# v's feature-major copy comes from memory, and only u is turned on the chip by a product with half an identity

## The chip, the cores and the metric

One core of one Trainium2 chip runs the whole program. The metric is the device time of one execution in microseconds (us). The engines are TensorE (PE, with its weight loads as PEld), VectorE (DVE), ScalarE (ACT), GpSimd (POOL) and SyncE (SP), which here issues all DMAs.

## What is computed

Inputs r, k, v, w, a, b of shape (4, 8, 768, 40), float32: 4 sequences, 8 heads, 768 time steps, 40 features. A state of 40 x 40 per head runs over time, and two dense layers follow on its 3072 x 320 outputs:

```
for t in range(S):
    y[:, :, t] = einsum('bhd,bhde->bhe', rt, state)
    Sa = einsum('bhde,bhe->bhd', state, at)
    state_decay = state * wt[:, :, None, :] - einsum('bhd,bhe->bhde', Sa, bt)
    state = state_decay + einsum('bhd,bhe->bhde', vt, kt)
x = (sigmoid(x @ w_gate) * (x @ w_val)) @ w_out          # x: y as 3072 x 320; hidden 1536
out = max(x @ w1, x @ w2, x @ w3) @ w_out2               # hidden 768
```

## The kernel before

**The recurrence.** Time is cut into 12 "pairs" (k = 0 to 11) of 64 steps. The heads stand in 12 slots of up to three heads (120 rows of features), in three groups g = 0, 1, 2 of four slots each: two parities (par) by two positions (pos). Groups 0 and 1 have slots of three heads (hd = 120), group 2 of two (hd = 80). Within a pair the updates of the state are solved as a triangular system: the grams of a (`ga`, six a pair, u = 2g + par) give its matrix, GpSimd inverts it for two pairs at once (`solve_block`, L385 to L400), and products with the inverse give u, the corrections of v. The tile `vu_rows` holds v and u with time on partitions: for each parity 64 rows of v at 64 * (1 - par) and 64 rows of u at 64 * par. From it come the state's increment (L495), and the grams of r (`gr`, L561), whose masked form (`gr_m`) times `kb_rows` gives y (L579).

The grams of r need v and u with features on partitions. That is the step `vt` (`turn_vu`, L517 to L525): four transposes a group on TensorE through the helper at L414 (all transposes stand under L415), each of 128 rows by hd columns, into the bank `p_tr`, which `ts` (the state) and `kb` also use in turn; ScalarE copies the result to `vu_t` (`keep_vu`, L804; all its copies stand under L752) and signals `tr_kept`.

**The order.** Every engine walks the same list of steps, `TURN` (L51 to L61), one turn a pair, with the pairs shifted against one another: in turn t, PE works on the solve of pair t, the outputs (`vt`, `gr`, `y`) of pair t - 1 and the grams of a of pair t + 3. In a turn the steps that matter here come in this order on PE:

```
vx 0, ga 0, ty 2, vt 0, ga 1, vx 1, t1 0, ga 2, ts 0, gr 0, ga 3, vx 2, t1 1, low 0, ga 4, gr 1, vt 1,
ga 5, y 0, t1 2, low 1, t2 0, gr 2, ts 1, ty 0, gr 3, low 2, t2 1, inc 0, vt 2, y 1, t2 2, kb 0, inc 1,
gr 4, ts 2, ty 1, gr 5, kb 1, inc 2, y 2, kb 2
```

Turns run from -4 to 13; `vt` stands in turns 1 to 12, `ga` in turns up to 8. The grams of a use one bank from pair 4 on, so each `ga` waits for VectorE's mask (`mask_a`, L667) of the one ahead; likewise each `gr` for `mask_r` (L676). In every even turn up to 8 VectorE turns the blocks of two pairs for the solve (`lab`, L682, behind `gr 2`), and at the end of every odd turn it turns the inverse (`inv`, L688), which it can do when GpSimd has finished; both stand in its order with everything else.

**The transfers.** SP issues every DMA in an order written out in its own `turn` (L280): in turn k the load of `r_m` (L265; r of one group, masked by head) for group 2 of pair k - 1, for group 0 and then group 1 of pair k, each behind the grams that used its buffer two groups before; the stores of y (L274, L277); and the loads of w, a, kb, v, r. Behind turn 11 SP first issues the loads of the next layer (`gated.load_x`, `gated.load_weights`, L881 to L949) and only then turn 12, with the last `load_rm(11, 2)`. The next layer begins when all engines have met at the end of the block.

**The two layers** behind it are dense products on TensorE (L875, L1045, L1260), each float32 operand split in a high and a low part.

Of the kernel before, what the change touches and what calls it, by code (L numbers as in the profile page):

```python
# [21 lines left out]
PT = 2 * C  # L22
PAIRS = SEQ // PT
SLOTS = 12
E3 = 120
# [4 lines left out]
GO = (0, 240, 480)  # L30
# [88 lines left out]
    return ap.broadcast_to(shape)  # L119


def recurrence(nc, w_in, a_in, kb_in, r_in, rm_in, v_in, x1_out, gated):
    ctx = ExitStack()
    with ctx:
        def sb(name, shape, dt=F32):
            return ctx.enter_context(nc.sbuf_tensor(name, shape, dt))

        def sem(name):
            return ctx.enter_context(nc.semaphore(name))
# [16 lines left out]
        a_m = sb("a_m", [E3, 2, 4, 3 * PT])  # L146
        r_t = sb("r_t", [E3, 2, SLOTS, PT])
        r_m = sb("r_m", [E3, 2, 4, 3 * PT])
        vu_t = sb("vu_t", [E3, 2, 4, 128])
        kb_rows = sb("kb_rows", [128, 5, 2, ROWS])  # L150
        vu_rows = sb("vu_rows", [128, 3, 2, ROWS])
        ak = sb("ak", [128, 4, 2, 16, PT])
# [14 lines left out]
        ld_w_first = sem("ld_w_first")  # L167
        ld_a = [sem(f"ld_a{x}") for x in range(5)]
        ld_v = [sem(f"ld_v{x}") for x in range(3)]
        ld_w, ld_kb, ld_r, ld_rm, st_y = ([sem(f"{n}{x}") for x in range(2)]  # L170
                                          for n in ("ld_w", "ld_kb", "ld_r", "ld_rm", "st_y"))
        consts = sem("consts")
        prod_done = sem("prod_done")
        ends_done = sem("ends_done")
# [35 lines left out]
        def w_of(k):  # L210

            if k == 1:
                return s_rows[:, :, :, :].rearrange("e z s f -> e (z s f)")[:, 0:4 * SLOTS * SEG].rearrange(
                    "e (z f) -> e z f", z=2)
            return w_raw

        def gram_bank(k, u):

# [7 lines left out]
        def _(sp):  # L226
# [33 lines left out]
            def load_rm(k, g):  # L260
                n = 3 * k + g
                if n >= 2:
                    sp.wait_ge(gr_done, 2 * (n - 2) + 2)
                rows, cols = HD[g], HPS[g] * PT
                sp.dma_start(r_m[0:rows, n % 2, :, 0:cols],  # L265
                             rm_in[k, 0:rows, 4 * g:4 * g + 4, 0:cols]).then_inc(ld_rm[n % 2], 16)

# [143 lines left out]
        def _(pe):  # L411
            mm = nc.tensor.matmul

            def turn(out, in_):  # L414
                return nc.tensor.transpose(out, in_, ident[0:in_.shape[0], 0:in_.shape[0]])  # L415
# [101 lines left out]
            def turn_vu(k, g):  # L517
                hd = HD[g]
                tr_free("vt", k, g)
                for par in range(2):  # L520
                    for pos in range(2):
                        at = 2 * par + pos
                        last = turn(p_tr[0:hd, at * 128:at * 128 + 128],
                                    vu_rows[:, k % 3, par, GO[g] + pos * hd:GO[g] + pos * hd + hd])
                last.then_inc(tr_done, 1)  # L525

            def turn_y(k, g):
# [23 lines left out]
            def gram_r(k, u):  # L551
                g, par = divmod(u, 2)
                n, hd, cols = 3 * k + g, HD[g], HPS[g] * PT
                if par == 0:
                    pe.wait_ge(tr_kept, TR_USE["vt", k, g] + 1)
                    pe.wait_ge(ld_rm[n % 2], 16 * (n // 2) + 16)
                pe.wait_ge(grm_done, 6 * k + u)
                if k == 0 and u == 0:
                    pe.wait_ge(akm_done, 24)
                for pos in range(2):  # L560
                    last = mm(p_gr[:, pos * cols:pos * cols + cols], vu_t[0:hd, n % 2, 2 * par + pos, :],  # L561
                              r_m[0:hd, n % 2, 2 * par + pos, 0:cols], start=pos == 0, stop=True,
                              skip_group_check=True)
                last.then_inc(gr_done, 1)
# [185 lines left out]
        def _(act):  # L750
            def copy(out, in_, scale=1.0):
                return nc.scalar.activation(out, in_, ACT.Copy, scale=scale)  # L752
# [51 lines left out]
            def keep_vu(k, g):  # L804
                n, hd = 3 * k + g, HD[g]
                act.wait_ge(tr_done, TR_USE["vt", k, g] + 1)
                if n >= 2:
                    act.wait_ge(gr_done, 2 * (n - 2) + 2)
                copy(vu_t[0:hd, n % 2, :, :], p_tr[0:hd, :].rearrange("e (s f) -> e s f", s=4)).then_inc(tr_kept, 1)

            def keep_y(k, g):
                n = 3 * k + g
# [559 lines left out]
            run_block(BLOCKS - 1, 1, False)  # L1372


def program(nc, w_in, a_in, kb_in, r_in, rm_in, v_in, w_gate, w_val, w_out, m_w1, m_w2, m_w3, m_out, out):
    x1 = nc.dram_tensor("x1", (BLOCKS, DM, BATCH, TB), F32).ap()
    with ExitStack() as ctx:

        lent_x = ctx.enter_context(nc.sbuf_tensor("lent_x", [128, 2 * SLOTS * 2 * SEG], F32))
        lent_w = ctx.enter_context(nc.sbuf_tensor("lent_w", [128, 2 * SLOTS * 128], F32))  # L1380
        gated = GatedInputs(nc, ctx, x1, w_gate, w_val, w_out, lent_x, lent_w)
        recurrence(nc, w_in, a_in, kb_in, r_in, rm_in, v_in, x1, gated)
        x2 = ctx.enter_context(nc.sbuf_tensor("x2", [128, BLOCKS, KT, TOK], F32))
        weights = MaxWeights(nc, ctx, (m_w1, m_w2, m_w3), m_out, lent_w)
        gated_layer(nc, gated, x2, weights)
        max_layer(nc, x2, weights, out.rearrange("(b n t) f -> n t b f", b=BATCH, n=BLOCKS))


def lay_out(r, k, v, w, a, b):
    def by_feature(x, pad):  # L1390
        out = np.full((PAIRS, E3, SLOTS, PT), pad, np.float32)
        for s, (bt, j) in enumerate(SLOT_HEADS):
            hs = x[bt, 3 * j:3 * j + 3]
            rows = hs.shape[0] * D
            out[:, 0:rows, s] = hs.reshape(-1, PAIRS, PT, D).transpose(1, 0, 3, 2).reshape(PAIRS, rows, PT)
        return out

    ws = by_feature(w, 1.0).reshape(PAIRS, E3, SLOTS, 2, C)
    w33 = np.zeros((PAIRS, E3, 2, SLOTS, 2, SEG), np.float32)
    w33[:, :, 0, :, :, 1:] = ws  # L1400
    w33[:, :, 1, :, :, 1:] = ws[..., ::-1]

    kf, bf = by_feature(k, 0.0), by_feature(b, 0.0)
    kb = np.zeros((PAIRS, E3, SLOTS, 2, PT), np.float32)
    rf = by_feature(r, 0.0)
    rm = np.zeros((PAIRS, E3, SLOTS, 3, PT), np.float32)
    vr = np.zeros((PAIRS, 2, PT, ROWS), np.float32)
    for s, (bt, j) in enumerate(SLOT_HEADS):
        g, par, pos = s // 4, s // 2 % 2, s % 2
        kb[:, :, s, 1 - par] = kf[:, :, s]  # L1410
        kb[:, :, s, par] = bf[:, :, s]
        for i in range(3):
            rm[:, i * D:(i + 1) * D, s, i] = rf[:, i * D:(i + 1) * D, s]
        hs = v[bt, 3 * j:3 * j + 3]
        cols = hs.shape[0] * D
        at = GO[g] + pos * HD[g]
        vr[:, par, :, at:at + cols] = hs.reshape(-1, PAIRS, PT, D).transpose(1, 2, 0, 3).reshape(PAIRS, PT, cols)
    return {
        "w_in": w33.reshape(PAIRS, E3, 2, SLOTS * 2 * SEG),
        "a_in": by_feature(a, 0.0),  # L1420
        "kb_in": kb.reshape(PAIRS, E3, SLOTS, 2 * PT),
        "r_in": rf,
        "rm_in": rm.reshape(PAIRS, E3, SLOTS, 3 * PT),
        "v_in": vr,
    }


# [15 lines left out]
```

## Time and profile before

| | us |
|---|---|
| median of 3 runs | 1127.23 |
| lowest, highest | 1122.25, 1128.94 |
| the profiled execution | 1123.35 |
| its span, first to last instruction | 1121.6 |
| PE busy in the span | 1039.6 (93%) |
| DVE, ACT, POOL busy | 514.6, 352.0, 291.3 |
| mean granted clock of TensorE | 0.954 of full speed |

A row of the timeline is a start, a length, the engine, the line, what was written from what, and how many instructions were merged; in brackets the idle time before it and what ended it. Granted clock 1.0 is 2.4 GHz, 0.5 is 1.2 GHz.

### The profile page before, as it was taken

The numbers are of one execution on the slowest core, as the hardware profiler recorded it, in microseconds if no ns is written. First come the engines' busy times: TensorE is split into PE (matmuls) and PEld (weight loads), VectorE is DVE, ScalarE is ACT, GpSimd is POOL, SyncE is SP. The second block draws the span as 40 slices with busy tenths as digits, with TensorE's granted clock in tenths as the row PEclk, the third lists the DMA queues.
The fourth block names the chain that finished last, engine by engine and source line by source line (L and its number), as shares of the span: only waits on it lengthen the run. The fifth ranks groups of instructions, "written<-read, shape, count | busy, mean of one in ns | idle before, by whom it ended". The sixth has DMA issues, their size and how long they took to land. (4 is left out here: it accounts for less than half of the span.)

```text
span 1121.6 us, 21667 instructions
## 1 busy us (share of the span) xinstructions
PE 1039.6 (93%) x8872; PEld 867.0 (77%) x8872; DVE 514.6 (46%) x875; ACT 352.0 (31%) x732; POOL 291.3 (26%) x527
## 2 busy tenths in 40 slices
PE   6577999899989996999999999999997999999998
PEld 3445778787778885788888888888885888888886
DVE  6726776567774443553323223332225543342432
ACT  3213544444444442432222222222223211111111
POOL 4788869588785500000000000000000000000000
PEclk7766999899999998899999999999998999999999
DMA  7632345455522225630000200000002100000000
GB/s 173 157 78 68 94 112 136 95 135 131 125 71 71 72 65 136 177 97 0 29 1 23 60 1 1 1 0 0 0 0 64 45 24 23 1 24 8 16 23 23
DMA packets 53247, 66.23 MB, mean 59 GB/s; under 512 B 19944, under 2 KB 40680, under 8 KB 53160
## 3 DMA queue, kind: packets, MB, share of 16 engines
q1 hardware_dynamic: 53160, 65.00, 22.7%
q8 instruction: 63, 1.03, 0.4%
q14 instruction: 24, 0.20, 0.1%
HBM read 57.12 MB, written 7.86 MB: 58 GB/s over the span
## 5 line engine op out<-in xcount | busy, mean ns | idle before, releaser
L1144 DVE TENSOR_TENSOR hid<-gate,gbank 128x512 f32<-128x512 f32 x72 | 49.5, 688 | 204.1 <-ACT gate L1090 204.1
L875 PE MATMUL mbank<-x_hi,w_hi 128*128 128x512 f32 x324 | 127.7, 394 | 6.7 <-DVE w_lo L1329 6.7
L392 POOL TENSOR_TENSOR inv_step<-lab 128x30 f32<-128x30 f32 (+9 forms) x180 | 120.0, 667 | 35.9 <-DVE lab L682 22.2
L875 PE MATMUL mbank<-x_hi,w_lo 128*128 128x512 f32 x324 | 127.0, 392 | 0.0
L1090 ACT ACTIVATE gate<-gbank 128x512 f32<-128x512 f32 x72 | 43.1, 598 | 226.4 <-PE gbank L875 226.4
L400 POOL TENSOR_TENSOR lab<-lab,inv_step 128x30 f32<-128x30 f32 (+9 forms) x180 | 110.4, 613 | 14.1
L1346 DVE TENSOR_TENSOR hid<-hid,mbank 128x512 f32<-128x512 f32 x72 | 49.5, 687 | 97.3 <-PE mbank L875 94.2
L875 PE MATMUL gbank<-x_hi,g_hi 128*128 128x512 f32 x216 | 84.9, 393 | 8.0 <-DVE v_lo L1124 8.0
L875 PE MATMUL mbank<-x_lo,w_hi 128*128 128x512 f32 x216 | 85.3, 395 | 0.0
L1045 PE MATMUL gbank<-h_hi,o_hi 128*128 128x512 f32 x216 | 84.1, 390 | 1.0 <-DVE h_lo L1150 1.0
L875 PE MATMUL gbank<-x_hi,g_lo 128*128 128x512 f32 x216 | 84.8, 392 | 0.0
L875 PE MATMUL gbank<-x_hi,v_hi 128*128 128x512 f32 x216 | 84.3, 391 | 0.0
L875 PE MATMUL gbank<-x_hi,v_lo 128*128 128x512 f32 x216 | 84.3, 390 | 0.0
L1045 PE MATMUL gbank<-h_lo,o_hi 128*128 128x512 f32 x216 | 84.0, 389 | 0.0
L546 PE MATMUL bank<-a_m,lent_w 120*128 120x192 f32 (+1 forms) x288 | 66.8, 371 | 18.2 <-DVE lent_w L657 10.9
L875 PEld LDWEIGHTS mbank<-x_hi,w_hi 128*128 128x128 f32 x324 | 61.5, 190 | 19.1 <-issue 7.1
L1150 DVE TENSOR_TENSOR h_lo<-hid,h_hi 128x512 fp32r<-128x512 f32 x72 | 49.9, 692 | 49.1 <-ACT h_hi L1095 49.1
L546 PEld LDWEIGHTS bank<-a_m,lent_w 120*128 120x128 f32 (+1 forms) x288 | 52.7, 224 | 24.7 <-issue 14.3
L875 PEld LDWEIGHTS mbank<-x_hi,w_lo 128*128 128x128 f32 x324 | 61.5, 190 | 13.2
L561 PE MATMUL bank<-r_m,vu_t 120*128 120x192 f32 (+1 forms) x288 | 59.5, 330 | 10.3 <-DVE gr_m L676 8.1
L752 ACT ACTIVATE b_sb<-bank 32x240 f32<-32x240 f32 x144 | 48.8, 339 | 63.3 <-PE bank L439 44.8
L374 POOL COPY lab_rows<-ak 32x192 f32<-32x192 f32 (+1 forms) x144 | 55.4, 384 | 40.6 <-DVE ak L667 34.6
(130 smaller groups left out, 2015.0 us busy)
## 6 DMA issues: line engine op xcount, KB each, us to landing
lent_w<-kb_in SPq DMA_DIRECT2D x12, 720.0 KB, 6.7
r_m<-rm_in SPq DMA_DIRECT2D x24, 360.0 KB, 3.7
lent_x<-w_in SPq DMA_DIRECT2D x10, 742.5 KB, 6.1
a_t<-a_in SPq DMA_DIRECT2D x12, 360.0 KB, 4.7
r_t<-r_in SPq DMA_DIRECT2D x11, 360.0 KB, 6.6
vu_rows<-v_in SPq DMA_DIRECT2D x24, 160.0 KB, 6.1
out<-o_sb SPq DMA_DIRECT2D x6, 640.0 KB, 3.2
x<-y_t SPq DMA_DIRECT2D x48, 60.0 KB, 3.2
```

The lines of the kernel that those rows point to most:

```text
L374: last = nc.gpsimd.tensor_copy(lab_rows[at:at + C, lane:lane + nh, :], ak[at:at + C, k % 4, par, HO[g]:HO[g] + nh, C * half:C * half + C])
L392: product = nc.gpsimd.tensor_tensor(part, column, row, op=ALU.mult)
L400: step(nc.gpsimd.tensor_tensor(rest, rest, part, op=ALU.subtract))
L546: last = mm(gram_bank(k, u)[:, pos * cols:pos * cols + cols], kb_t[0:hd, k % 2, slot_of(g, par, pos), :], a_m[0:hd, n % 2, 2 * par + pos, ...
L561: last = mm(p_gr[:, pos * cols:pos * cols + cols], vu_t[0:hd, n % 2, 2 * par + pos, :], r_m[0:hd, n % 2, 2 * par + pos, 0:cols], start=pos ...
L752: return nc.scalar.activation(out, in_, ACT.Copy, scale=scale)
L875: last = mm(out, w, x, start=n == 0, stop=n == len(seq) - 1)
L1045: last = nc.tensor.matmul(p_out[t][:, :], w, h, start=m == 0 and n == 0, stop=m == M1 - 1 and n == len(seq) - 1)
L1090: nc.scalar.activation(gate[:, m % 2, :], p_gate[m % 2][:, :], ACT.Sigmoid).then_inc(gate_done, 1)
L1144: nc.vector.tensor_tensor(hid[:, m % 2, :], gate[:, m % 2, :], p_val[m % 2][:, :], op=ALU.mult).then_inc(hid_done, 1)
L1150: nc.vector.tensor_tensor(h_lo[:, m % 2, :], hid[:, m % 2, :], h_hi[:, m % 2, :].bitcast(F32), op=ALU.subtract).then_inc(hl_done, 1)
L1346: nc.vector.tensor_tensor(hid[:, n, m % 2, :], hid[:, n - 1, m % 2, :], bank_of(b, m, n)[:, :], op=ALU.max).then_inc(most, 1)
```

## The change

The host gives v a second time, as `vt_in`, in the layout by features that a and r have. SP loads of it, ahead of each load of `r_m` and behind the same wait, the two slots of each parity straight into `vu_t`, where v's half of the 128 columns lies: 2 loads a group, 72 in all, of 120 (or 80) rows by 2 runs of 256 bytes. On TensorE `turn_vu` no longer transposes all 128 rows. It takes an ordinary product of the same weights (128 rows by hd columns of `vu_rows`) with 64 columns of the identity, those of u's rows, so that 64 columns come out; ScalarE copies 4 x 64 columns instead of 4 x 128 into u's places in `vu_t`. The grams of r wait for the two loads too (`ld_vt`). `vu_t` grows from 512 to 640 elements a buffer so that one slice can name u's places of both parities.

```diff
-        vu_t = sb("vu_t", [E3, 2, 4, 128])
+        vu_t = sb("vu_t", [E3, 2, 5 * 128])
...
+        def vu_slots(n, par):
+
+            return vu_t[:, n % 2, 256 * par:256 * par + 256].rearrange("e (o t) -> e o t", o=2)
...
                 if n >= 2:
                     sp.wait_ge(gr_done, 2 * (n - 2) + 2)
                 rows, cols = HD[g], HPS[g] * PT
+                for par in range(2):
+                    at = slot_of(g, par, 0)
+                    sp.dma_start(vu_slots(n, par)[0:rows, :, 64 * (1 - par):64 * (1 - par) + 64],
+                                 vt_in[k, 0:rows, at:at + 2, :]).then_inc(ld_vt[n % 2], 16)
                 sp.dma_start(r_m[0:rows, n % 2, :, 0:cols],
                              rm_in[k, 0:rows, 4 * g:4 * g + 4, 0:cols]).then_inc(ld_rm[n % 2], 16)
...
                 for par in range(2):
                     for pos in range(2):
                         at = 2 * par + pos
-                        last = turn(p_tr[0:hd, at * 128:at * 128 + 128],
-                                    vu_rows[:, k % 3, par, GO[g] + pos * hd:GO[g] + pos * hd + hd])
+                        last = mm(p_tr[0:hd, at * PT:at * PT + PT],
+                                  vu_rows[:, k % 3, par, GO[g] + pos * hd:GO[g] + pos * hd + hd],
+                                  ident[:, 64 * par:64 * par + 64], start=at == 0, stop=True, skip_group_check=True)
                 last.then_inc(tr_done, 1)
...
                     pe.wait_ge(ld_rm[n % 2], 16 * (n // 2) + 16)
+                    pe.wait_ge(ld_vt[n % 2], 32 * (n // 2) + 32)
...
-                    last = mm(p_gr[:, pos * cols:pos * cols + cols], vu_t[0:hd, n % 2, 2 * par + pos, :],
+                    last = mm(p_gr[:, pos * cols:pos * cols + cols], vu_slots(n, par)[0:hd, pos, :],
...
-                copy(vu_t[0:hd, n % 2, :, :], p_tr[0:hd, :].rearrange("e (s f) -> e s f", s=4)).then_inc(tr_kept, 1)
+                u_part = vu_t[0:hd, n % 2, :].rearrange("e (p x) -> e p x", p=2)[:, :, 0:256].rearrange(
+                    "e p (o x) -> e p o x", o=2)[:, :, :, 0:PT]
+                copy(u_part, p_tr[0:hd, 0:4 * PT].rearrange("e (p o x) -> e p o x", p=2, o=2)).then_inc(tr_kept, 1)
...
+        "vt_in": by_feature(v, 0.0),
```

## Rows read from the trace of the kernel before

**Rows 1.** Busy time by stretches of 40 us: PE, PEld, DVE, ACT, POOL, clock, DMA.

```profile
280.00:320.00 40.00, 36.91 (x656) 31.20 (x655) 27.64 (x55) 19.02 (x48) 31.11 (x48) 1.00 0.43 103
...
560.00:1121.00 561.00, 548.64 (x2556) 463.19 (x2554) 194.48 (x275) 129.38 (x216) 0.00 (x0) 0.99 0.06 17
```

**Rows 2.** Timeline of VectorE, the turns of lower blocks and inverse, 283 to 387 us.

```profile
284.12 1.94 DVE L682 STREAM_TRANSPOSE lab<-lab_rows 128x1024 f32<-128x1024 f32 x1
...
330.91 1.97 DVE L688 STREAM_TRANSPOSE inv_rows<-lab 128x1024 f32<-128x1024 f32 x1 [1.19 <-POOL lab L400]
...
346.52 1.93 DVE L682 STREAM_TRANSPOSE lab<-lab_rows 128x1024 f32<-128x1024 f32 x1
...
383.38 1.95 DVE L688 STREAM_TRANSPOSE inv_rows<-lab 128x1024 f32<-128x1024 f32 x1
```

**Rows 3.** Timeline of PE in turn 12, grams of group 2.

```profile
438.01 0.68 PE L561 MATMUL bank<-r_m,vu_t 80*128 80x128 f32 x4 [1.36 <-issue]
```

**Rows 4.** Timeline of SP's queue, turns 11 and 12.

```profile
425.30 0.35 SPq L265 DMA_DIRECT2D r_m<-rm_in  x1
425.69 0.90 SPq L274 DMA_DIRECT2D x<-y_t  x2
...
427.20 1.18 SPq L941 DMA_DIRECT2D lent_x<-x  x2
...
429.06 2.35 SPq L883 DMA_DIRECT2D lent_w<-moe_w_gate  x2
...
434.55 0.61 SPq L265 DMA_DIRECT2D r_m<-rm_in  x1
...
446.19 0.41 SPq L881 DMA_DIRECT2D x<-moe_w_gate  x1
```

**Rows 5.** PE's groups by shape, 0 to 450 us: busy us, mean ns, idle.

```profile
L579 PE MATMUL bank<-kb_rows,gr_m 128*64 128x40 f32 x768 | 28.6, 228 | 0.1
L495 PE MATMUL bank<-vu_rows,kb_rows 128*120 128x120 f32 x176 | 23.4, 276 | 4.0 <-DVE s_t L703 3.2 <-issue 0.7
...
L415 PE MATMUL bank<-ident,vu_rows 128*80 128x128 f32 x48 | 7.2, 273 | 0.0
...
L415 PE MATMUL bank<-ident,s_t 80*80 80x80 f32 x44 | 4.8, 233 | 0.0
```

**Rows 6.** Timeline of PE about "vt 0" and "vt 1".

```profile
300.73 0.60 PE L415 MATMUL bank<-ident,vu_rows 128*120 128x128 f32 x4
301.42 0.89 PE L546 MATMUL bank<-a_m,lent_w 120*128 120x192 f32 x4
...
310.75 0.60 PE L415 MATMUL bank<-ident,vu_rows 128*120 128x128 f32 x4
311.19 0.61 PE L546 MATMUL bank<-a_m,lent_w 80*128 80x128 f32 x4
```

**Rows 7.** Timeline of PE, the products used as prices.

```profile
318.73 1.00 PE L495 MATMUL bank<-vu_rows,kb_rows 128*120 128x120 f32 x8
...
320.56 0.85 PE L579 MATMUL bank<-kb_rows,gr_m 128*64 128x40 f32 x24
...
329.53 0.50 PE L415 MATMUL bank<-ident,lent_w 80*128 80x80 f32 x4 [0.88 <-ACT kb_rows L752]
```

**Rows 8.** ScalarE's groups by shape: busy us, mean ns, idle.

```profile
L752 ACT ACTIVATE vu_t<-bank 120x512 f32<-120x512 f32 x24 | 14.3, 597 | 21.6 <-PE bank L415 21.5
L752 ACT ACTIVATE y_rows<-bank 128x240 f32<-128x240 f32 x24 | 8.9, 370 | 18.8 <-PE bank L579 18.8
```

**Rows 9.** Timeline of a usual turn: r_m of group 2 issued, then used.

```profile
310.95 0.34 SPq L265 DMA_DIRECT2D r_m<-rm_in  x1
...
323.86 0.62 PE L561 MATMUL bank<-r_m,vu_t 80*128 80x128 f32 x4
```

**Rows 10.** DMA issues: count, KB each, us from issue to landing.

```profile
r_m<-rm_in SPq DMA_DIRECT2D x24, 360.0 KB, 3.7
```

**Rows 11.** Busy time in one stretch, columns as in rows 1.

```profile
207.00:214.00 7.00, 7.00 (x57) 6.09 (x54) 1.51 (x3) 2.44 (x6) 2.36 (x8) 0.52 0.35 73
```

More of the change, by code:

```diff
@@ L119, in bc, with recurrence @@
     return ap.broadcast_to(shape)
-def recurrence(nc, w_in, a_in, kb_in, r_in, rm_in, v_in, x1_out, gated):
+def recurrence(nc, w_in, a_in, kb_in, r_in, rm_in, v_in, vt_in, x1_out, gated):
     ctx = ExitStack()
@@ L169, in recurrence @@
         ld_v = [sem(f"ld_v{x}") for x in range(3)]
-        ld_w, ld_kb, ld_r, ld_rm, st_y = ([sem(f"{n}{x}") for x in range(2)]
-                                          for n in ("ld_w", "ld_kb", "ld_r", "ld_rm", "st_y"))
+        ld_w, ld_kb, ld_r, ld_rm, ld_vt, st_y = ([sem(f"{n}{x}") for x in range(2)]
+                                          for n in ("ld_w", "ld_kb", "ld_r", "ld_rm", "ld_vt", "st_y"))
         consts = sem("consts")
@@ L1372, in _, with program @@
             run_block(BLOCKS - 1, 1, False)
-def program(nc, w_in, a_in, kb_in, r_in, rm_in, v_in, w_gate, w_val, w_out, m_w1, m_w2, m_w3, m_out, out):
+def program(nc, w_in, a_in, kb_in, r_in, rm_in, v_in, vt_in, w_gate, w_val, w_out, m_w1, m_w2, m_w3, m_out, out):
     x1 = nc.dram_tensor("x1", (BLOCKS, DM, BATCH, TB), F32).ap()
@@ L1381, in program @@
         gated = GatedInputs(nc, ctx, x1, w_gate, w_val, w_out, lent_x, lent_w)
-        recurrence(nc, w_in, a_in, kb_in, r_in, rm_in, v_in, x1, gated)
+        recurrence(nc, w_in, a_in, kb_in, r_in, rm_in, v_in, vt_in, x1, gated)
         x2 = ctx.enter_context(nc.sbuf_tensor("x2", [128, BLOCKS, KT, TOK], F32))
```

## The prediction

> **What bounds the kernel now.** I read the page first (one core, TensorE, called PE, is the busiest engine), then the table by stretches of 40 us [rows 1]. The change touches only the recurrence, which ends near 446 us; behind 560 us PE is busy for 548.6 of 561 us, at a granted clock of 0.99, in the two layers that the diff leaves alone. Inside the recurrence PE is busy for 92% of a middle stretch (280 to 320), but a busy share does not say which wait sets the pace, so I looked in the timeline for waits that close a loop.
>
> There is one. In every second turn VectorE turns the inverse for two pairs (L688), and it stands idle before it until GpSimd has finished its solve (L400): 1.19 us at 330.91 [rows 2], and waits of the same kind stand in turns 2, 4 and 6. The solve can start only when VectorE has turned the lower blocks (L682, at 284.12 and 346.52), and from the end of that turn (284.12 + 1.94 = 286.06) to L688 GpSimd needs 44.8 us [rows 2]. So a period of two turns, 346.52 - 284.12 = 62.4 us, has two parts. From L682 to L688, 46.8 us, GpSimd sets the pace, and PE has 1.19 us to spare. From L688 to the next L682, some 15.6 us, PE does. After 346.52 nothing more is solved for later: L688 at 383.38 stands without idle, PE is in front to the end, and its work counts in full.
>
> The last stretch is different again. In turn 12 PE stands still for 1.36 us before the grams of group 2 (438.01) [rows 3] and the releaser is "issue", which is no engine. Before that the queue of SP works through a backlog: from 425.30 to 435 one transfer follows another, because the loads of the next layer stand between the loads of r_m. The last r_m is issued at 434.55 and PE goes on 3.46 us later [rows 3, 4]. I read this as the wait for that transfer.
>
> **What the change removes, adds and moves.** There are 36 steps "vt" (12 pairs by 3 groups). Each was four transposes of all 128 rows of vu_rows, and becomes four products with 64 columns of the identity.
>
> *PE.* The transposes of group 2 have 48 records, one for each of 12 x 4 [rows 5]. An ordinary float32 product leaves two: L495 has 176 records at groups 0 and 1, where the program has 11 x 2 x 4 = 88 products [rows 5]. So the four new products are eight passes of 64 columns, against four of 128: the same number of columns. The pitch of a transpose is (600 - 273) / 3 = 109 ns (four in 0.60 us, one lasting 273 ns) [rows 5, 6], so a step is 436 ns now. For a product pass of 120 columns, eight in 1.00 us give (1000 - 276) / 7 = 103 ns [rows 5, 7]; that is 0.86 ns a column, 55 ns for 64. Is the weight load hidden beneath 55 ns? At L579, 24 passes take 0.85 us, two by two in two halves of the array: (850 - 228) / 23 = 27 ns each, 54 ns for a pair that loads 2 x 64 = 128 columns and streams only 40 [rows 5, 7]. So 54 ns are a load of about 128 columns, and 120 columns hide just under the stream. With two to spare I take 57 ns, 8 x 57 = 456 ns, 20 ns more than now. Below, 53 ns (8 x 53 = 424, 12 ns less); above, the 4 turns of 80 columns with weights 128 wide, which take at most (500 - 233) / 3 = 89 ns each [rows 5, 7]: 8 x 89 = 712, 276 ns more. The row nearest in width and kind is L495, which is why I stay low.
>
> The Trainium skill, "TensorE: Matmul & The Clock Gate", section "LDWEIGHTS (loading the stationary operand)", prices a load at its columns over 1.2, so 100 ns for 120 columns; each step would then be an estimated 8 x 100 = 800 ns. The trace disagrees: 54 ns for 128 columns at L579.
>
> Which steps count? "vt 0" of turns 1 to 8 is followed by a gram of a that waits for the mask of the gram ahead; PE is idle there: four transposes from 300.73 have streamed at 300.73 + 0.44 = 301.17, and the next product starts at 301.42 [rows 6]. 20 ns vanish in those 0.25 us. "vt 1" (310.75) is followed at once, 0.44 us later, by the next gram (311.19) [rows 6], and "vt 2" by outputs, so they move PE. But only what lies between L688 and L682 (vt 1 of turns 2, 4, 6, 8: 4 steps) or behind the last L682 (vt 2 of turn 8 and three steps in each of turns 9 to 11: 10 steps) moves the end. The rest is taken from PE's 1.19 us to spare. 14 x 0.020 = +0.28 us; at the two ends 14 x (-0.012) = -0.2 and 14 x 0.276 = +3.9 us.
>
> *ScalarE.* The copy of a step goes from 512 to 256 elements a row. 597 ns for 512 and 370 for 240 from PSUM [rows 8] are 0.83 ns an element, so 383 ns: 214 ns less, 36 times. Nothing waits for it until turn 12: after "vt" PE uses the same bank again only two or more steps later, and the grams that read vu_t come turns or half turns on. In turn 12 the first gram does wait for it, but what that gains stands before the 1.36 us of idle and is lost in them. Worth nothing.
>
> *The transfers.* 72 loads of 60 or 40 KB in runs of 256 bytes; the stores of y have that shape and cost SP 0.45 us each (two in 0.90) [rows 4]. In a usual turn there is cover: r_m of group 2 is issued at 310.95 and used at 323.86 [rows 9], 12.9 us for two more issues (0.9) and 3.7 us of landing [rows 10]. If that cover went, "gr" would wait and y behind it. The added wait itself (PE on ld_vt) is one more semaphore among four on the same step and ends before the gram is due.
>
> Not so in turn 12. Each load of r_m now has two loads of v ahead of it on SP, and SP is the one that is late. Two stand at 425.30, behind the last gram of turn 11 that frees the buffer: 0.85 us, the first short issue (0.35) and one of the usual. Two more stand before 434.55 in the backlog, where two short transfers take 1.18 us [rows 4]: 1.2 us. Together 2.05 us, by which the last r_m lands later, counted from the end of turn 11. PE waits for it already, so it all goes to the end: y of the last group, its turn, its store, and the next layer, which starts when all engines have met (SP's first load there at 446.19) [rows 4]. Bounds: 4 x 0.33 = 1.3 us if each cost the shortest issue shown (0.35), 3.2 us if the backlog stalls once more as at 429.06 (2.35 for two instead of 1.18).
>
> **The sum.** 0.28 + 2.05 = +2.3 us. Against the profiled span, 1121.6 + 2.3 = 1123.9 us. That execution took 1123.35 us in all, 1.75 more than its span, and the median of the runs is 1127.23, their spread 6.7 us. So I predict 1127.2 + 2.3 = 1129.5 us. What a measurement of this kernel can tell from no change is about 1%, 11.3 us.
>
> **The rivals.**
> *The last r_m is not what PE waits for, or SP's extra issues hide.* For it: "issue" names no transfer. Against it: nothing else of that step is late. Then +0.3 us: 1127.5.
> *The clock gains.* PE's granted clock falls to 0.52 (about the lower level, 1.2 of 2.4 GHz) from 207 to 214 us and is back at 1.00 behind it [rows 11]. That stretch lies behind L688, where PE counts. At half clock 6.8 us do the work of 3.4, so without it the end is up to 3.4 us earlier: 1129.5 - 3.4 = 1126.1. The Trainium skill, same page, "Part 4: PE-mode transpose", says that full speed does not engage for a transpose; products in their place would then help. In this trace transposes at full clock stand everywhere (109 ns), and no row singles them out.
> *The weight loads do not hide,* 100 ns a pass: 800 - 436 = 364 ns a step, 14 times, 5.1 us, and within a period 3 x 0.36 + 0.11 = 1.2 us just uses up PE's 1.19. 1127.2 + 5.1 + 2.05 = 1134.4. Against it: L579.
> *The other side: the clock loses.* The longer wait at 438 and the fuller queue let the clock fall more often. It decides only from (11.3 - 2.3) x 2 = 18 us more at half clock where PE sets the pace, almost three stretches like that of 207 to 214. Then 1127.2 + 2.3 + 10.2 = 1139.7. Nothing in the change lengthens an idle time in the usual turns, so I hold it unlikely.
>
> **How the numbers follow.** Forecast 0.56, no effect 0.13, clock gains 0.13, loads do not hide 0.10, clock loses 0.06, a gain that I don't see 0.02. The first four lie from 1126 to 1134.4; with the runs' own spread about each median (3 us down, 2 up) the range is 1123 to 1136. Faster by over 1% 0.02, within 1% 0.91, slower by over 1% 0.07.
>
> **What would show it.** In the profile after: 288 records of 128x64 at the new product, eight in about 0.63 us (pitch 57 ns); the copy near 383 ns; L688 still idle behind GpSimd, the period still 62.4 us; PE's idle before the grams of group 2 of turn 12 up from 1.36 to about 3.3 us; SP's first load of the next layer about 2.3 us after 446.19. I am wrong if a product leaves one record of 64 columns (then a step saves 0.2 us and the total about 3 us), if the period changes, or if the idle in turn 12 stays.

## The result and the profile after

| | before | after |
|---|---|---|
| median, us | 1124.74 | 1137.36 |
| lowest, highest | 1120.83, 1128.94 | 1134.16, 1138.08 |
| profiled execution, its span | 1123.35, 1121.6 | 1137.60, 1135.9 |
| mean granted clock | 0.954 | 0.953 |

The ratio is 1.0087 (95% interval 1.0051 to 1.0123): slower by about 10 us, where 2.3 were forecast. (The ratio comes with its interval from the measurement and is not the quotient of the two medians, which lie 12.6 us apart.) Two later sittings of the same pair gave 1.0032 (1.0001 to 1.0063) and 1.0077 (1.0059 to 1.0095). All three are under the 1% or so that the prediction took as the least that can be told from no change, but each interval lies wholly above 1. The median of the first, 1137.36 us, lies 1.4 us above the top of my range.

First the groups that changed. PE's and ScalarE's groups by shape, kernel after (busy us, mean ns, idle); the first three answer to [rows 5], the fourth to [rows 8]:

```profile
L531 PE MATMUL bank<-ident,vu_rows 128*120 128x64 f32 x192 | 23.7, 268 | 0.0
L531 PE MATMUL bank<-ident,vu_rows 128*80 128x64 f32 x96 | 8.7, 234 | 0.0
L503 PE MATMUL bank<-vu_rows,kb_rows 128*120 128x120 f32 x176 | 23.4, 276 | 4.4 <-DVE s_t L713 4.0 <-issue 0.5
...
L762 ACT ACTIVATE vu_t<-bank 120x256 f32<-120x256 f32 x24 | 9.2, 384 | 27.9 <-PE bank L531 27.9
```

192 + 96 = 288 records of 128x64, two for each product, and a copy of 384 ns: both as forecast. What is not as forecast is how fast the passes follow each other. Timeline of PE, kernel after, about "vt 1" and "vt 2" (the first pair answers to [rows 6]), then "vt 2" before:

```profile
315.36 0.96 PE L531 MATMUL bank<-ident,vu_rows 128*120 128x64 f32 x8
316.15 0.66 PE L555 MATMUL bank<-a_m,lent_w 80*128 80x128 f32 x4
...
323.92 0.72 PE L531 MATMUL bank<-ident,vu_rows 128*80 128x64 f32 x8
324.57 0.63 PE L585 MATMUL bank<-s_rows,r_t 120*64 120x120 f32 x8
```

```profile
319.57 0.60 PE L415 MATMUL bank<-ident,vu_rows 128*80 128x128 f32 x4
320.10 0.63 PE L575 MATMUL bank<-s_rows,r_t 120*64 120x120 f32 x8
```

From the start of the step to the start of what follows: 0.44 us before [rows 6] and 0.79 after with 120 weight columns, +0.35; 0.53 and 0.65 with 80, +0.12. Forecast was +0.02 for either. From record to record most passes start 105 ns (120 columns) or 71 to 72 ns (80) after the last, not 57, though both stream the same 64 columns.

Next, the hand-overs between GpSimd and PE. VectorE's timeline, turns of lab and inv, kernel before (the five that [rows 2] does not show), and kernel after:

```profile
93.48 1.95 DVE L682 STREAM_TRANSPOSE lab<-lab_rows 128x1024 f32<-128x1024 f32 x1 [2.13 <-POOL lab_rows L374]
140.54 1.95 DVE L688 STREAM_TRANSPOSE inv_rows<-lab 128x1024 f32<-128x1024 f32 x1 [2.97 <-POOL lab L400]
156.13 1.94 DVE L682 STREAM_TRANSPOSE lab<-lab_rows 128x1024 f32<-128x1024 f32 x1
202.93 1.94 DVE L688 STREAM_TRANSPOSE inv_rows<-lab 128x1024 f32<-128x1024 f32 x1 [2.52 <-POOL lab L400]
221.69 1.95 DVE L682 STREAM_TRANSPOSE lab<-lab_rows 128x1024 f32<-128x1024 f32 x1
```

```profile
93.90 1.95 DVE L692 STREAM_TRANSPOSE lab<-lab_rows 128x1024 f32<-128x1024 f32 x1 [2.14 <-POOL lab_rows L382]
143.07 1.94 DVE L698 STREAM_TRANSPOSE inv_rows<-lab 128x1024 f32<-128x1024 f32 x1
160.02 1.96 DVE L692 STREAM_TRANSPOSE lab<-lab_rows 128x1024 f32<-128x1024 f32 x1
207.22 1.94 DVE L698 STREAM_TRANSPOSE inv_rows<-lab 128x1024 f32<-128x1024 f32 x1 [2.52 <-POOL lab L408]
226.35 1.96 DVE L692 STREAM_TRANSPOSE lab<-lab_rows 128x1024 f32<-128x1024 f32 x1
...
289.53 1.96 DVE L692 STREAM_TRANSPOSE lab<-lab_rows 128x1024 f32<-128x1024 f32 x1
336.74 1.94 DVE L698 STREAM_TRANSPOSE inv_rows<-lab 128x1024 f32<-128x1024 f32 x1 [2.52 <-POOL lab L408]
355.89 1.93 DVE L692 STREAM_TRANSPOSE lab<-lab_rows 128x1024 f32<-128x1024 f32 x1
393.69 1.94 DVE L698 STREAM_TRANSPOSE inv_rows<-lab 128x1024 f32<-128x1024 f32 x1
```

At 143.07 the bracket with POOL is gone: there GpSimd is no longer what VectorE waits for. The differences of these starts (with inv at 273.56 after and 268.47 before) are the parts of the recurrence. "Solve n" runs from lab to inv, "hand-over n" from inv to lab, "tail" from the fifth lab (346.52 before, 355.89 after) to the last inv, "end" from there to the first product of the next layer (451.13 before, 465.67 after).

| part | before | after | difference |
|---|---|---|---|
| up to the first lab | 93.48 | 93.90 | +0.4 |
| solve 1 | 47.06 | 49.17 | +2.1 |
| hand-over 1 | 15.59 | 16.95 | +1.4 |
| hand-over 2 | 18.76 | 19.13 | +0.4 |
| hand-over 3 | 15.65 | 15.97 | +0.3 |
| hand-over 4 | 15.61 | 19.15 | +3.5 |
| solves 2, 3, 4 | 46.80, 46.78, 46.79 | 47.20, 47.21, 47.21 | +1.2 |
| tail | 36.86 | 37.80 | +0.9 |
| end | 67.75 | 71.98 | +4.2 |
| sum | | | +14.5 |

Last, turn 12. PE's timeline, kernel after: a gram of r of turn 11, and that of the last group (this one answers to [rows 3]); then SP's queue (to [rows 4]):

```profile
435.33 0.71 PE L571 MATMUL bank<-r_m,vu_t 80*128 80x128 f32 x4
...
452.54 0.68 PE L571 MATMUL bank<-r_m,vu_t 80*128 80x128 f32 x4 [3.26 <-DMA r_m<-rm_in]
```

```profile
437.30 0.83 SPq L271 DMA_DIRECT2D vu_t<-vt_in  x2
438.17 1.50 SPq L273 DMA_DIRECT2D r_m<-rm_in  x1
...
447.34 1.16 SPq L271 DMA_DIRECT2D vu_t<-vt_in  x2
448.54 0.44 SPq L273 DMA_DIRECT2D r_m<-rm_in  x1
...
460.73 0.40 SPq L893 DMA_DIRECT2D x<-moe_w_gate  x1
```

The idle time rose from 1.36 to 3.26 us and now names the transfer; 3.3 was forecast. The gram at 435.33 starts 41.64 us behind the last inv; before it stood at 423.33, 39.95 us behind. So 1.7 us of the 4.2 in the end are PE's own in turns 10 and 11, and 2.5 are SP's.

### The profile page after: what moved, and what is told of

Read it like the earlier page. It is cut to its first block and busy times, and to the rows that moved or that the text cites. A ratio compares the mean times of both kernels' runs of the same rounds, so it can differ in the third digit from the quotient of the medians.

```text
span 1135.9 us, 22062 instructions
## 1 busy us (share of the span) xinstructions
PE 1052.7 (93%) x9016; PEld 884.6 (78%) x9016; DVE 512.3 (45%) x875; ACT 344.5 (30%) x732; POOL 293.4 (26%) x527
## 5 line engine op out<-in xcount | busy, mean ns | idle before, releaser
L1156 DVE TENSOR_TENSOR hid<-gate,gbank 128x512 f32<-128x512 f32 x72 | 49.5, 687 | 204.3 <-ACT gate L1102 204.3
L1358 DVE TENSOR_TENSOR hid<-hid,mbank 128x512 f32<-128x512 f32 x72 | 49.4, 687 | 97.2 <-PE mbank L887 94.1
L555 PE MATMUL bank<-a_m,lent_w 120*128 120x192 f32 (+1 forms) x288 | 67.8, 376 | 19.1 <-DVE lent_w L667 10.7
L887 PEld LDWEIGHTS mbank<-x_hi,w_hi 128*128 128x128 f32 x324 | 61.5, 190 | 19.1 <-issue 7.1
L555 PEld LDWEIGHTS bank<-a_m,lent_w 120*128 120x128 f32 (+1 forms) x288 | 53.9, 228 | 23.9 <-issue 13.5
L1162 DVE TENSOR_TENSOR h_lo<-hid,h_hi 128x512 fp32r<-128x512 f32 x72 | 49.8, 692 | 49.1 <-ACT h_hi L1107 49.1
L382 POOL COPY lab_rows<-ak 32x192 f32<-32x192 f32 (+1 forms) x144 | 58.3, 405 | 47.9 <-DVE ak L677 42.0
L762 ACT ACTIVATE b_sb<-bank 32x240 f32<-32x240 f32 x144 | 48.9, 340 | 68.6 <-PE bank L447 50.9
```

The costliest lines, as they stand in the source:

```text
L382: last = nc.gpsimd.tensor_copy(lab_rows[at:at + C, lane:lane + nh, :], ak[at:at + C, k % 4, par, HO[g]:HO[g] + nh, C * half:C * half + C])
L555: last = mm(gram_bank(k, u)[:, pos * cols:pos * cols + cols], kb_t[0:hd, k % 2, slot_of(g, par, pos), :], a_m[0:hd, n % 2, 2 * par + pos, ...
L887: last = mm(out, w, x, start=n == 0, stop=n == len(seq) - 1)
L1156: nc.vector.tensor_tensor(hid[:, m % 2, :], gate[:, m % 2, :], p_val[m % 2][:, :], op=ALU.mult).then_inc(hid_done, 1)
L1162: nc.vector.tensor_tensor(h_lo[:, m % 2, :], hid[:, m % 2, :], h_hi[:, m % 2, :].bitcast(F32), op=ALU.subtract).then_inc(hl_done, 1)
L1358: nc.vector.tensor_tensor(hid[:, n, m % 2, :], hid[:, n - 1, m % 2, :], bank_of(b, m, n)[:, :], op=ALU.max).then_inc(most, 1)
```

## The experiments

Theory A: an ordinary float32 pass lasts as long as the load of its weights, if that is longer than its stream. Theory B, that of the forecast: the stream sets the pace, and the loss beyond 2.3 us is the clock's or the transfers'. All kernels in one table, ratios to before with 95% intervals; parts in us from each profiled execution, with before and after repeated.

| kernel | ratio | solve 1 | hand-overs 1, 2, 3, 4 | tail | end |
|---|---|---|---|---|---|
| before | | 47.1 | 15.6, 18.8, 15.7, 15.6 | 36.9 | 67.7 |
| e1 loads only | 1.0024 (0.9993 to 1.0054) | 47.2 | 15.6, 18.7, 15.6, 15.6 | 36.9 | 69.4 |
| e6 before, last r_m early | 0.9978 (0.9948 to 1.0009) | 47.4 | 18.7, 18.7, 15.6, 18.8 | 36.9 | 65.2 |
| e13 the same again | 0.9984 (0.9963 to 1.0006) | 47.3 | 20.1, 18.7, 15.6, 15.6 | 36.9 | 65.1 |
| e8 loads only, early | 0.9979 (0.9948 to 1.0009) | 47.1 | 15.6, 18.8, 18.7, 15.6 | 36.9 | 66.0 |
| e10 after, transposes kept | 1.0047 (1.0024 to 1.0069) | 47.1 | 15.6, 18.8, 18.7, 15.6 | 36.9 | 70.2 |
| e11 the same, early | 0.9978 (0.9957 to 1.0000) | 47.2 | 20.1, 18.7, 15.6, 18.8 | 36.9 | 66.9 |
| after | 1.0087 (1.0051 to 1.0123) | 49.2 | 16.9, 19.1, 16.0, 19.1 | 37.8 | 72.0 |
| e4 after again | 1.0032 (1.0001 to 1.0063) | 48.9 | 17.0, 16.0, 16.0, 16.0 | 37.8 | 72.3 |
| e12 after, a third time | 1.0077 (1.0059 to 1.0095) | 49.4 | 17.0, 19.2, 16.0, 19.2 | 37.8 | 71.1 |
| e2 after, no loads | 1.0047 (1.0019 to 1.0076) | 49.5 | 17.0, 16.0, 17.0, 16.0 | 37.8 | 68.5 |
| e5 after, early | 1.0059 (1.0032 to 1.0087) | 49.1 | 16.9, 19.1, 16.0, 19.1 | 37.8 | 67.9 |
| e3 products of 128 columns | 1.0008 (0.9978 to 1.0038) | 47.4 | 19.2, 16.0, 16.0, 16.5 | 38.6 | 69.4 |
| e9 transposes twice | 1.0004 (0.9971 to 1.0038) | 47.4 | 19.2, 16.0, 16.1, 16.0 | 38.6 | 69.3 |

**The loads alone (e1).** Ahead of each r_m load in the kernel before (shown without the tile and TensorE's wait):

```diff
+                for par in range(2):
+                    at = slot_of(g, par, 0)
+                    sp.dma_start(vt_x[0:rows, n % 2, par, :].rearrange("e (o t) -> e o t", o=2),
+                                 vt_in[k, 0:rows, at:at + 2, :]).then_inc(ld_vt[n % 2], 16)
```

> The kernel before with the 72 loads of v with features on partitions added ahead of each r_m load, into a spare tile that nothing reads; TensorE waits for them in front of the grams of r as in the changed kernel, and the transposes and the copy stay as they were. Theory SP: these loads cost only at turn 12, where four of their issues stand ahead of the last r_m: the idle time in front of the last group's gram of r grows from 1.36 us [rows 3] to 3.3 us or somewhat more, and the median rises by 2 to 2.5 us (ratio 1.0018 to 1.0022); every hand-over of lab and inv up to the eleventh turn stands within 0.5 us of before. Rival, loads cost bandwidth or queue time everywhere: the hand-overs drift apart from the first turns on, and the median rises by 5 us or more. Rival, the loads bring the longer stretches of half clock: then this kernel shows them too (one of 7 us behind 336 us).

1129.80 us, ratio 1.0024. Every part up to the last inv is that of before within 0.1 us. PE's timeline in turn 12:

```profile
439.12 0.68 PE L567 MATMUL bank<-r_m,vu_t 80*128 80x128 f32 x4 [3.31 <-DMA r_m<-rm_in]
```

The last r_m is issued 53.2 us behind the last inv (435.76 - 382.56), against 51.17 before (434.55 - 383.38): 2.03 us later, where I had worked out 2.05. The end is 1.7 us longer. So in the parts the 72 loads cost nothing but at this one place; the interval of the total reaches below 1 and could not show it.

**The products alone (e2).** The loads after the first two groups are left out:

```diff
-                for par in range(2):
+                for par in range(2 if n < 2 else 0):
...
-                    pe.wait_ge(ld_vt[n % 2], 32 * (n // 2) + 32)
+                    pe.wait_ge(ld_vt[n % 2], 32)
```

> The changed kernel without its loads of v after the first two groups (left out: from the third group on the grams of r read, for v's half of the tile, what those first loads brought); TensorE's products with half an identity and ScalarE's narrower copy stay. Theory weight load: a pass of the product lasts as long as the load of its 120 or 80 weight columns (105 and 71.5 ns in the trace of after), so vt takes 840 ns where it took 436 and 570 where it took 436; the idle time at the last group's gram of r is back near 1.36 us, the hand-overs of lab and inv drift as in after (+0.3 to +0.4 us in each part from inv to lab, about +0.9 us in the part of lab 8, some +0.8 us in each of turns 10 and 11), and the median stands 5 to 10 us over before, the upper part of it only if the longer stretches of half clock come with the products. Theory stream (that of my forecast, 57 ns a pass): at most 1 us over before, and the rest of the 12.6 us was in the loads.

1133.79 us, ratio 1.0047. Tail 37.8, undisturbed hand-overs 16.0, solve 1 at 49.5 us: all of after's, without a load. That rules theory B out. The idle time at the last gram is 0.61 us; I had expected 1.36, but PE comes there 2.3 us later than before by its own work (55.6 us behind the last inv against 53.3), and the wait ends only 1.6 us later (56.2 against 54.6).

**Twice the stream, same weights (e3).** In the kernel before:

```diff
-                        last = turn(p_tr[0:hd, at * 128:at * 128 + 128],
-                                    vu_rows[:, k % 3, par, GO[g] + pos * hd:GO[g] + pos * hd + hd])
+                        last = mm(p_tr[0:hd, at * 128:at * 128 + 128],
+                                  vu_rows[:, k % 3, par, GO[g] + pos * hd:GO[g] + pos * hd + hd],
+                                  ident[:, :], start=at == 0, stop=True, skip_group_check=True)
```

> The kernel before with one edit: the four transposes of v and u become ordinary products with the whole identity, so 128 columns stream instead of the 64 of the changed kernel, with the same weights (120 or 80 columns); no loads of v, the copy stays 512 wide. Theory weight load: a pass takes the longer of load and stream, so about 109 ns at 120 weight columns and also about 109 ns at 80 (stream of 128 columns): vt about 870 ns in all three groups, and the median is 5 to 12 us over before, near the changed kernel, though twice as much streams. Theory stream: a pass of 128 columns costs twice one of 64, so this kernel loses some 6 us more than the changed one does in its products.

PE's timeline, "vt 1" and "vt 2":

```profile
313.74 1.04 PE L523 MATMUL bank<-ident,vu_rows 128*120 128x128 f32 x8
314.62 0.61 PE L547 MATMUL bank<-a_m,lent_w 80*128 80x128 f32 x4
...
322.33 1.04 PE L523 MATMUL bank<-ident,vu_rows 128*80 128x128 f32 x8
323.30 0.63 PE L576 MATMUL bank<-s_rows,r_t 120*64 120x120 f32 x8
```

Most passes start 109 ns after the last at 120 weight columns and at 80. With after's numbers this makes a square: 64 streamed columns 105 and 72 ns, 128 streamed columns 109 and 109. At 120 weight columns doubling the stream costs 4 ns; at 80 it costs 37. The longer of the two sets the pass; theory A holds for ordinary products. Transposes with wide weights don't follow it: the four of 80 rows by 128 columns in [rows 7] start at most 89 ns apart, in the trace mostly 69, less than the 105 ns of a product with only 120 weight columns. Why is not tested. The price goes through as it should: step +0.44 us for each group, tail 38.60 - 36.86 = 1.74 us, which is four steps (4 x 0.44 = 1.76). But the total that I expected, 5 to 12 us, is missed: 1129.53 us, ratio 1.0008. Below I return to that.

**Each transpose twice (e9).**

```diff
-                        last = turn(p_tr[0:hd, at * 128:at * 128 + 128],
-                                    vu_rows[:, k % 3, par, GO[g] + pos * hd:GO[g] + pos * hd + hd])
+                        for again in range(2):
+                            last = turn(p_tr[0:hd, at * 128:at * 128 + 128],
+                                        vu_rows[:, k % 3, par, GO[g] + pos * hd:GO[g] + pos * hd + hd])
```

> The kernel before with each of the four transposes of v and u issued twice over (the second writes the same result): 8 passes of 128 columns as in the kernel with products by the whole identity, but transposes. Theory: the pass price is the stream's, 109 ns, so vt takes about 870 ns in all groups and every hand-over of lab and inv stands as in that kernel (0.4 us more in each part from inv to lab, first product of the next layer 6 to 7 us later than before). On the clock: if it is the products that shorten the stretches of half clock (some 85 us in that kernel against 100 before), this kernel keeps the 100 us of before and comes out 6 us over it; if it is the mere streaming of more columns, it has some 85 us too and comes out 1 to 3 us over before.

1128.21 us, ratio 1.0004, passes of 109 ns, and parts like those of e3 to 0.1 us but for one hand-over. So a product that streams 128 columns brings nothing that two transposes don't.

**The changed kernel with the last loads early (e5).**

```diff
-                if 1 <= k <= PAIRS:
+                if 1 <= k < PAIRS:
...
+            load_rm(PAIRS - 1, 2)
             sp.wait_ge(kbt_done, 2 * PAIRS)
```

> The changed kernel with one move: the last group's loads of r_m and v are issued right behind turn 11, ahead of SP's wait for the transposed kb and ahead of the first loads of the next layer, instead of in turn 12. Theory SP: the idle time of 3.26 us in front of the last group's gram of r goes to nothing that the load causes, and the median falls by 2 to 3.3 us against the changed kernel (1137.36 us), to about 1134.5 us, ratio to before about 1.0065. If the next layer's first load were what sets the end instead, the median does not fall, since that load then starts later.

1133.10 us, against 1137.36 in after, 1137.35 in e12 and 1129.84 in e4: the sittings of the changed kernel lie on both sides of it, so the total decides nothing, and only the part shows the gain. The end falls from 71.1 to 72.3 us in the three of them to 67.9, by 3.2 to 4.4 us, where 2 to 3.3 were expected of the median.

**The changed kernel again (e4, e12).**

> The changed kernel once more, on the chip and in the rounds of the runs beside it, to have its distance from before beside theirs. If the two parts add up (loads alone +2.4 thousandths, products alone +4.7 thousandths of before), the ratio comes out at 1.007 to 1.008; if the products and the loads together bring something that neither brings alone (their longer stretches of half clock, or a GpSimd part of 47.2 us in place of 46.8), at 1.009 or more.

> The changed kernel a third time, since its distance from before came out at 9 and at 3 thousandths in two sittings. Theory clock: each part from inv to lab takes 16.0 us, or 19.1 where a stretch of half clock falls on it, and executions differ by how many of the four are hit; so the ratio lies between the two, 1.005 to 1.008, and the profile again has 48.9 to 49.2 us in the second part from lab to inv with a stretch of half clock of 24 us behind lab. Rival, the chips differ: then it falls on one of the two values again.

1129.84 and 1137.35 us. VectorE's timeline of e4 at the fourth hand-over:

```profile
330.72 1.97 DVE L698 STREAM_TRANSPOSE inv_rows<-lab 128x1024 f32<-128x1024 f32 x1 [2.04 <-POOL lab L408]
346.74 1.95 DVE L692 STREAM_TRANSPOSE lab<-lab_rows 128x1024 f32<-128x1024 f32 x1
```

16.0 us, where after has 19.15 (336.74 to 355.89). PE and the clock behind that inv, columns as in [rows 1], first after, then e4:

```profile
340.00:347.00 7.00, 7.00 (x71) 6.41 (x71) 1.65 (x4) 2.45 (x6) 3.09 (x10) 0.53 0.07 15
```

```profile
334.00:341.00 7.00, 7.00 (x150) 6.26 (x150) 3.02 (x6) 3.70 (x10) 3.74 (x12) 1.00 0.08 16
```

PE is busy in both, but at half clock it does 71 matmuls where it does 150 at full. [rows 11] is the same thing at hand-over 2 of before. So a hand-over lasts 15.6 us (16.0 with the products), or 3.1 more when a stretch of half clock of 6.8 us falls on it, and 4.5 more with one of 13.7 us (e11, e13). (The trace keeps the granted clock as a list of stretches at one level; I call them the clock records.) The number of hand-overs hit differs between the profiles of one kernel: none in e4, two in after and e12; one in the profile of before and in e1, two in e5, e8, e10 and e13, three in e6 and e11. After and e4 differ by 8.8 us in their parts; two hits more are 6.2 of these, GpSimd's solves 1.4, and the time up to the first lab 1.3. So the hits are most of the gap between the sittings, as far as one profile of each tells. What decides them is open: five of e4's six executions took 1127.7 to 1131.1 us and one 1136.5, the ten of after and e12 all 1134.2 to 1138.3. That looks like a matter of the sitting more than of the single execution, and the rival named for e12, that chips differ, is not ruled out.

**The kernel before with the last r_m early (e6, e13).** The same move as in e5.

> The kernel before with one move: the last group's load of r_m is issued right behind turn 11, ahead of SP's wait for the transposed kb and of the next layer's first loads. Theory SP: the idle time of 1.36 us in front of the last group's gram of r [rows 3] goes, and the time falls by about that, to a ratio of 0.9985 to 0.999, a version faster than both kernels if little. Rival: the next layer's first loads, which now stand behind it, or what holds the end of the recurrence besides, take the gain back and the ratio is 1.000.

> The kernel before with its last r_m load early, once more in these rounds, to narrow its distance from before. Theory SP: inv to the next layer's first product takes 65.2 us again where it took 67.7, which makes a ratio of 0.9978, if as many parts are hit by half clock as in before; with the two sittings together, below 1.000.

1125.15 us and 1126.00 us (before beside them: 1127.45 and 1127.43). PE's timeline:

```profile
442.01 0.71 PE L562 MATMUL bank<-r_m,vu_t 80*128 80x128 f32 x4
```

No bracket: the idle time is gone. The gram stands 53.2 us behind the last inv (442.01 - 388.81), 1.4 less than before, as its 1.36 of idle said; the end is 2.6 us shorter. The other 1.1 us lie behind the gram, where the stretch of half clock lasts 10.2 us and not 17.1 (clock records). Both intervals still reach above 1.000, so faster is likely, not shown. That the shorter half clock made the 1.1 us is read off these profiles (e13 has 10.2 us and an end of 65.1 too), not tested by itself.

**Loads only, early (e8).** e1 and e6 together.

> The kernel before with the 72 added loads of v into a spare tile, and with the last group's loads (v's and r_m) issued right behind turn 11, as in the kernel that moves r_m alone. Theory SP: the added loads cost only where they delay the last r_m, so with that load out of the way they cost nothing: the idle time in front of the last gram of r is gone and the time equals that of the kernel before with the early r_m, ratio 0.9985 to 0.9995. Rival, the loads cost something in every turn: the ratio stays at 1.001 or above.

1125.67 us, ratio 0.9979, the same as e6: with the last r_m out of the way, the loads cost nothing that the total shows. The end is 0.8 us longer than e6's (66.0 against 65.2), with PE waiting 8.9 us for VectorE before the next layer's first product where it waits 8.0 in e6.

**The changed kernel with the transposes kept (e10), and early (e11).**

```diff
-                        last = mm(p_tr[0:hd, at * PT:at * PT + PT],
-                                  vu_rows[:, k % 3, par, GO[g] + pos * hd:GO[g] + pos * hd + hd],
-                                  ident[:, 64 * par:64 * par + 64], start=at == 0, stop=True, skip_group_check=True)
+                        last = turn(p_tr[0:hd, at * 128:at * 128 + 128],
+                                    vu_rows[:, k % 3, par, GO[g] + pos * hd:GO[g] + pos * hd + hd])
```

(The parities change places in the bank and the tile, so that one narrow copy still takes u's half.)

> The changed kernel with one part undone: v still comes from memory and ScalarE still copies only u's half, but u is turned by the four transposes of before (436 ns in a step) instead of the eight product passes. Theory weight load: the whole price of the products goes, so the parts are those of the kernel with the loads alone: inv to lab 15.6 us where no half clock falls on it (16.0 with the products), 36.9 us for the last part (37.8), lab to inv 47.2 us for the second part (48.9 to 49.5), the stretch of half clock behind 94 us 17 us long (24 with the products), inv to the next layer's first product 69.4 us or up to 0.5 less for the narrower copy (72 with the products); ratio to before 1.001 to 1.0025. Rival, the narrower copy or the loads into the tile that is read bring the longer stretch: the second part stays at 48.9 us or more.

> The same kernel (v from memory, transposes kept, narrow copy) with the last group's loads issued right behind turn 11. Theory: nothing is left that costs, so it stands with the kernel before that has its last r_m early, or 0.2 to 0.5 us below it for the narrower copy: inv to the next layer's first product 65 to 66 us, ratio to before 0.997 to 0.9985. It would be the best version of the change's idea, and should be faster than both kernels.

e10: 1131.45 us, ratio 1.0047; e11: 1126.32 us, ratio 0.9978. In the parts, undoing the products alone takes off all that theory A lays on them: hand-overs 15.6, tail 36.9, solve 1 47.1. PE at half clock shows the last of these. The window 112 to 122 us, columns as in [rows 1], in before, after, e2 and e10, one fence each:

```profile
112.00:122.00 10.00, 10.00 (x211) 8.88 (x211) 6.07 (x10) 5.08 (x14) 9.06 (x13) 1.00 0.21 56
```

```profile
112.00:122.00 10.00, 10.00 (x80) 8.84 (x79) 2.07 (x4) 2.83 (x7) 8.90 (x15) 0.50 0.01 2
```

```profile
112.00:122.00 10.00, 10.00 (x80) 8.99 (x80) 2.13 (x5) 2.83 (x7) 8.84 (x14) 0.50 0.01 3
```

```profile
112.00:122.00 10.00, 10.00 (x201) 8.88 (x203) 6.04 (x10) 4.67 (x14) 9.01 (x12) 1.00 0.18 48
```

The clock records say the same for all: behind the first lab half clock lasts 23.9 us in every profile with products of 64 columns (after, e2, e4, e5, e12), 13.7 to 17.1 us in every other. It costs some 2 us in solve 1 and 1 us in hand-over 1. Still, e10's ratio is above the 1.001 to 1.0025 expected; its interval meets that of e1, and I can't tell the two apart. Its end is 0.7 us longer than e1's, with a half clock of 20.5 us there. Its median is 5.9 us below that of the changed kernel beside it (e12), though the two intervals still overlap.

e11 was to be faster than both kernels. It is 5.1 us below e10 and its interval against before reaches 1.0000, but it stands level with e6 and e13 (0.9978, 0.9984), which take nothing from the change but the early r_m. So with both of its costs taken away, v from memory and the narrower copy gain nothing that these runs can tell.

## Why the forecast was wrong

**The price of a pass: the step that failed.** I took 57 ns for a product pass and 20 ns a step; it is 105 or 72 ns, and 350 or 120 ns a step. It failed at the reading of L579 in [rows 7]. I took 54 ns for a load of 128 columns, since two loads of 64 stand in two halves of the array. They run side by side (in the trace the two records of a pair start 7 ns apart and the next pair 51 or 52 ns later), so 54 to 59 ns are the load of 64. That puts a load at 0.84 to 0.92 ns a column, and 105 and 72 ns at 120 and 80 columns are 0.88 and 0.90. The other row I stayed close to, L495, has 120 columns on both sides, so it can't show which of them sets its 103 ns. I had dismissed the right value: the Trainium skill, "TensorE: Matmul & The Clock Gate", section "LDWEIGHTS (loading the stationary operand)", gives columns over 1.2, 100 ns for 120 and 67 for 80; the trace agrees with 4 to 5 ns on top. "The weight loads do not hide", with 1134.4 us and a chance of 0.10, was the case that came true, for its mechanism: its 364 ns for every step are 350 and 120, and its total lacks what the clock added. My upper bound of 276 ns a step also lay below the truth at 120 columns. That the result still stayed within 1%, as I gave 0.91 for, is luck: my price of a pass was off by nearly half, and the loss it left out happened to be small beside the whole.

**Which steps count: right.** By the rows of the steps, 4 x 0.35 in the hand-overs, 0.12 in turn 8 and 0.82 in each of turns 9 to 11 are 4.0 us. Measured, leaving out what half clock adds: 0.3 to 0.4 in each hand-over, 1.5 in all, 0.9 in the tail, 1.7 in turns 10 and 11, together 4.1.

**What bounds the period: right.** GpSimd still ends the solves 2, 3 and 4, and in e4, where it takes 46.7 us for them, what the steps within a solve cost PE stays within its time to spare. The period itself is 62.7 us there (283.96 - 221.22) and not 62.4, by the one step in the hand-over.

**ScalarE's copy: right in length and worth.** 384 ns, and e10, which has it without the products, gains nothing in sum.

**Turn 12: right.** 2.05 forecast for the delay of the last r_m; 2.03 us in e1, where the end grew by 1.7, and 2.5 us of the end in after. The rival by which the last r_m is not what PE waits for falls with e1 and e6.

**The clock: a rival with the wrong sign, and the part left out.** I wrote that nothing in the change lengthens an idle time in the usual turns and priced the clock at nothing. The 64-column products bring 7 to 10 us more of half clock behind the first lab, some 3 us of time, in all five profiles; e10 shows that it is the products. How the 3 us divide between solve 1 and hand-over 1 is my reading, and why the products keep the clock down longer is open. What I also did not see is that the profile of before stood for one throw of several: half clock can fall on none to three hand-overs.

So the 14.5 us between the two profiled executions are 4.1 for the products at full clock, 2.5 for SP in turn 12, about 3.1 for the longer half clock behind the first lab (2.1 in solve 1 and 1.0 of hand-over 1), 3.1 for a second hand-over that was hit here and not in the profile of before, 1.2 in GpSimd's solves and 0.4 before the first lab. The first three, 9.7 us, belong to the change and are about the 9 to 10 us of the sittings at 1.0087 and 1.0077; e2 and e1 alone, 4.7 and 2.4 thousandths, add to 8.0 us.

**Open.** e3 and e9 lay more work on PE than after does (tail 38.6) and yet come out level with before. Their mean granted clock is the highest of all (0.962 and 0.964 over their runs, 0.954 and 0.956 for before beside them), and in their profiles one hand-over was hit in full, against two on average in the seven profiles with four transposes a step (one to three). That fits, but that hand-overs are hit less often there was counted in one profile each, and not tested. GpSimd's solves of 47.2 us in after, in e5 and in two of three in e12, against 46.7 to 46.8 in e4 and before, are not explained; they don't belong to the change alone, since single solves of 47.3 us stand in e8, e10, e11 and e13 too. (In e2 one solve took 50.9 us with half clock on it.)

## What to carry to other kernels

Price an ordinary float32 product at two passes, each the longer of its weight load (0.88 ns a weight column at full clock, as measured at 120 columns and about so at 80) and its stream; halving the streamed columns of a product whose stationary operand is wide saves next to nothing (109 to 105 ns a pass at 120), and a transpose, which needs one pass, is then the cheaper way to turn a tile. Take the price of a pass only from a row in which load and stream differ, and look whether it fills the array or half of it. Before a change's time is read off one pair of profiles, cut both into the same parts and take out those that a stretch of half clock happened to hit.

## What the runs showed of the hardware

- Two loads of 64 weight columns into the two column halves of the array run side by side: 54 to 59 ns for the pair, where 120 columns in one piece take 105.
- With an idle time of 1.4 us gone before the end of the recurrence (e6), the half clock behind it lasted 10.2 us in place of 17.1, and the end was 2.6 us shorter; in the changed kernel, with 3.3 us of idle gone (e5), it lasted 13.7 in place of 17.1, and the end was 4 us shorter.
- Transposes issued twice (e9) and products of the same shape (e3) went with a like rise of the mean granted clock, to 0.964 and 0.962 from 0.956 and 0.954. The Trainium skill, "TensorE: Matmul & The Clock Gate", section "Part 4: PE-mode transpose", has it that full clock does not engage for transposes; these runs don't bear that out, with transposes 109 ns apart at full clock. So the rival "the clock gains" lost its ground, and no run of the changed kernel shows such a gain.
- Products with 64 streamed columns in the place of transposes went with 23.9 us of half clock behind the first lab in five profiles of five; with transposes or with 128 streamed columns it was 13.7 to 17.1 us in nine of nine.
